# A gated linear attention in chunks with two dense layers: the alpha check per chunk, a reordered prologue, and TensorE's tile loop written out

## The reference, cut to what matters

```python
B, H, S, D = 4, 8, 768, 48
for t in range(S):                                  # per batch and head
    state = alpha[:, :, t, :, None] * state + k[t] (outer) v[t]
    y[:, :, t] = q[t] @ state                       # D x D state
x = y.transpose(0, 2, 1, 3).reshape(3072, 384)
x = (1 / (1 + exp(-(x @ w_gate))) * (x @ w_val)) @ w_out        # 384 -> 1536 -> 384
x = max(max(x @ w1, x @ w2), x @ w3) @ w_out2                   # 384 -> 768 -> 384
```

## Time and profile before

| what | us |
|---|---|
| median of 3 executions (892.06 to 894.14) | 893.74 |
| the profiled execution, its own time | 890.85 |
| its span, first to last instruction | 889.1 |
| TensorE busy in the span | 855.4 (96%) |
| VectorE, ScalarE, POOL busy | 413.7, 263.2, 120.8 |
| TensorE's mean granted clock | 0.989 |

### The profile page before, as it was taken

The page is one execution under the profiler, slowest core; times in us unless marked ns, Lnnn a source line. Parts: engine busy times, 40 slices in busy tenths (PEclk is TensorE's granted clock), DMA queues, the critical chain, the costliest instruction groups (busy, mean ns, idle before and its releaser), DMA issues.

```text
span 889.1 us, 13943 instructions
## 1 busy us (share of the span) xinstructions
PE 855.4 (96%) x5405; PEld 797.8 (90%) x5405; DVE 413.7 (47%) x730; ACT 263.2 (30%) x502; POOL 120.8 (14%) x95
## 2 busy tenths in 40 slices
PE   4599999999989999989999999999999999999997
PEld 3499999999989999989999999988888888888886
DVE  7888466366356456555546532232323222232321
ACT  3535333233232332232232233421212222121311
POOL 4355411011011111101101102510000000000000
PEclk9789999999999999999999999999999999999999
DMA  7481021021021021021021021300010000000000
GB/s 298 140 330 46 7 90 46 8 90 46 6 93 45 1 96 45 1 97 45 1 97 45 1 78 32 111 1 1 0 36 1 35 0 35 0 35 0 18 18 35
DMA packets 15603, 46.89 MB, mean 53 GB/s; under 512 B 2112, under 2 KB 6080, under 8 KB 15552
## 3 DMA queue, kind: packets, MB, share of 16 engines
q1 hardware_dynamic: 15552, 46.15, 14.7%
HBM read 40.24 MB, written 4.72 MB: 51 GB/s over the span
## 4 chain that ended last, share of the span: by engine, by line
PE 94%; DVE 2%; issue 1%; ACT 1%; DMA 1%; POOL 0%; SPq 0%; ACTq 0%; DVEq 0%; POOLq 0%
PE ps_gate L799 17%; PE ps_out L824 17%; PE ps_val L799 17%; PE ps_gate L805 8%; PE ps_val L805 8%; PE ps_out L896 6%; PE ps_sc L799 6%; PE ps_sc L805 3%; PE ps_sc L757 3%; PE ps_y L788 3%; PE ps_sc_odd L896 2%; PE ps_y L784 2%; PE ps_y L741 1%; PE ps_sc L767 1%; DVE rdec L566 1%
## 5 line engine op out<-in xcount | busy, mean ns | idle before, releaser
L799 PE MATMUL ps_gate<-x_hi,w_hi 128*128 128x384 f32 (+1 forms) x396 | 139.8, 353 | 7.2 <-issue 5.4
L799 PE MATMUL ps_val<-x_hi,w_hi 128*128 128x384 f32 (+1 forms) x396 | 140.7, 355 | 0.0
L799 PE MATMUL ps_gate<-x_hi,w_lo 128*128 128x384 f32 (+1 forms) x396 | 139.1, 351 | 0.0
L799 PE MATMUL ps_val<-x_hi,w_lo 128*128 128x384 f32 (+1 forms) x396 | 138.9, 351 | 0.0
L805 PE MATMUL ps_gate<-x_lo,w_hi 128*128 128x384 f32 (+1 forms) x396 | 118.1, 352 | 0.0
L629 DVE TENSOR_TENSOR h_sb<-act_sb,ps_val 128x384 f32<-128x384 f32 x96 | 52.7, 549 | 139.9 <-PE ps_val L805 139.8
L805 PE MATMUL ps_val<-x_lo,w_hi 128*128 128x384 f32 (+1 forms) x396 | 117.2, 350 | 0.0
L387 ACT ACTIVATE h_hi<-h_sb 128x384 fp32r<-128x384 f32 x96 | 50.4, 525 | 156.7 <-DVE h_sb L629 156.6
L428 ACT ACTIVATE act_sb<-ps_gate 128x384 f32<-128x384 f32 x96 | 47.2, 492 | 157.2 <-PE ps_gate L805 156.8
L714 DVE TENSOR_TENSOR probs<-probs,ps_val 128x512 f32<-128x512 f32 x36 | 24.7, 687 | 137.8 <-PE ps_val L805 137.8
L566 DVE RECIPROCAL rdec<-decay 112x128 f32<-112x128 f32 x96 | 85.7, 923 | 0.5
(11 more groups left out here) (98 smaller groups left out, 1245.7 us busy)
## 6 DMA issues: line engine op xcount, KB each, us to landing
inbuf<-att_in SPq DMA_DIRECT2D x23, 704.0 KB, 5.2
mid<-w SPq DMA_DIRECT2D x12, 576.0 KB, 9.3
inbuf<-att_in SPq DMA_DIRECT2D x23, 256.0 KB, 3.0
mid<-alpha_flat SPq DMA_DIRECT2D x8, 576.0 KB, 7.2
inbuf<-w SPq DMA_DIRECT2D x6, 768.0 KB, 4.3
out<-inbuf SPq DMA_DIRECT2D x5, 768.0 KB, 3.5
x_raw<-y_last SPq DMA_DIRECT2D x48, 24.0 KB, 1.9
out<-inbuf SPq DMA_DIRECT2D x4, 192.0 KB, 2.1
```

Of the source, the lines that this page charges most:

```text
L799: mm(bank, w_at(half, f, c + k * P, total=total), x_hi[:, k, 0:w], start=(k == 0 and half == 0), stop=False)
```

## The change

Every chunk's alpha is checked where it lies, after its scans, on ScalarE (two passes: |alpha - 1|, then relu(that - 0.25) with its row sum into a column of `viol`). The flag is made from the 24 columns in tile 7 and read by every engine after all its other work; the general path, now with both layers in it, follows there. `alpha_flat`, `distance`, `reduce_alpha`, the clamp, `finish_x` and its register are gone. `rdec` is no longer a reciprocal of `decay`: the last column is, and a second scan multiplies backwards from it by alpha. The prologue has another order on every engine. TensorE's loop over two tiles is written out as six tiles; the other engines keep theirs.

```diff
 def load_chunk(Cs, i):                                  # SP
     if isinstance(i, int) and Cs in (3, 4):
         sp.wait_ge(y_done, 5 - Cs)
+        sp.wait_ge(viol_done, 5 - Cs)
     elif not (isinstance(i, int) and Cs < 3):
         sp.wait_ge(u_done, Cs + 6 * i - 1)
+        sp.wait_ge(viol_done, Cs + 6 * i - 1)
...
+def load_w1(f):
+    if f >= RING:
+        sp.wait_ge(w_hi_done, f - RING + 1)
+        sp.wait_ge(w_lo_done, f - RING + 1)
+    elif f >= RING - 2:
+        sp.wait_ge(y_done, 3)
+        sp.wait_ge(viol_done, 3)
+    sp.dma_start(slot(f), w1[f]).then_inc(stage_in[f % RING], 16)
...
 load_chunk(0, 0)
+load_chunk(1, 0)
 sp.dma_start(cst[:, :], consts).then_inc(consts_in, 16)
-load_chunk(1, 0)
-load_ring(0)
-load_ring(1)
+load_w1(0)
 load_chunk(2, 0)
...
+for f in range(1, RING - 2):
+    load_w1(f)
+load_chunk(4, 0)
+load_chunk(3, 0)
+move_last(0, (0, 2))
+for f in range(RING - 2, NF1):
+    load_w1(f)
+load_chunk(5, 0)
+move_last(1)
```

POOL splits `w1[0]` in three parts, and TensorE's first gate and val product wait for a part each:

```diff
 scale_qk(0, 0)
 scale_qk(1, 0)
-split_w1(0)
+split_first(0).then_inc(w_lo_part, 1)
 scale_qk(2, 0)
-for f in range(1, NF1):
-    split_w1(f)
+split_first(1).then_inc(w_lo_part, 1)
+split_first(2).then_inc(w_lo_done, 1)
+for f in range(NF1):
+    if f > 0:
+        split_w1(f)
     if f in (2, 5, 8):
         scale_qk(CPT + (f - 2) // 3, 0)
```

ScalarE (`y_copy` now copies `y_last` first and signals it; `check` comes in every tile's f = 2, 5, 8 after h_hi):

```diff
+def check(Cs, i):
+    C = Cs + 6 * i
+    act.wait_ge(rdec_done, C * PAIRS + PAIRS)
+    a = buf_cols(buf(Cs), 0, PAIRS * CH)
+    nc.scalar.activation(a, a, ACT.Abs, bias=minus_one).then_inc(dist_done, 1)
+    act.wait_ge(dist_done, C + 1)
+    col = viol[:, bass.ds(C, 1)]
+    nc.scalar.activation(a, a, ACT.Relu, bias=minus_range, accum_out=col).then_inc(viol_done, 1)
...
+khs_copy(0, 0)
 split_w1(0)
-distance(0)
-khs_copy(0, 0)
-distance(1)
+act.wait_ge(consts_in, 16)
 y_copy(0, 0)
-distance(2)
 khs_copy(1, 0)
-split_w1(1)
-distance(3)
+check(0, 0)
+check(1, 0)
 y_copy(1, 0)
...
 y_copy(2, 0)
-for n in range(7, NA):
-    distance(n)
-split_w1(2)
+act.wait_ge(last_evac, CPT)
+for r in (0, ODD):
+    act.dma_start(x_raw[r + D:r + D + GAP, 1, :],
+                  y_last[r + GAP:r + 2 * GAP, :]).then_inc(last_moved[1], 16)
+khs_copy(2, 0)
+split_w1(1)
+act.wait_ge(y_evac, CPT)
 for k in range(KT):
     act.wait_ge(last_moved[k], 32)
     x_split(0, k, x_raw[:, k, :])
-act.wait_ge(flag_ready, 1)
-bad = act.value_load(flag_i[0:1, 0:1], min_val=0, max_val=1)
...
-layer1(0, 0, True, False, {f: (lambda f=f: split_w1(f + 3)) for f in range(NF1 - 3)})
+layer1(0, 0, True, False, {f: after_first_tile(f) for f in range(NF1 - 2)})
```

where `after_first_tile(f)` makes `check(2, 0)` at f = 0 and then `split_w1(f + 2)`. VectorE:

```diff
 def recips(Cs, i, pairs):
+    C, par = Cs + 6 * i, Cs % 2
+    if 0 in pairs:
+        dve.wait_ge(scan_done, C * PAIRS + PAIRS)
...
+        nc.vector.reciprocal(rdec[0:PR, par, :, CH - 1], decay[0:PR, par, :, CH - 1]).then_inc(rend_done, 1)
+        nc.vector.tensor_copy(d_end[0:PR, par, :], decay[0:PR, par, :, CH - 1]).then_inc(end_done, 1)
+        dve.wait_ge(rend_done, C + 1)
     for p in pairs:
-        nc.vector.reciprocal(rdec[0:PR, Cs % 2, p, :], decay[0:PR, Cs % 2, p, :]).then_inc(rdec_done, 1)
+        nc.vector.tensor_tensor_scan(rdec[0:PR, par, p, CH - 2::-1], att(buf(Cs), ALPHA)[:, p, CH - 1:0:-1],
+                                     zero[0:PR, :].broadcast_to([PR, CH - 1]), rdec[0:PR, par, p, CH - 1:CH],
+                                     ALU.mult, ALU.add).then_inc(rdec_done, 1)
...
-dve.wait_ge(consts_in, 16)
 scans(0, 0)
 recips(0, 0, range(PAIRS))
 scans(1, 0)
+recips(1, 0, range(PAIRS))
+dve.wait_ge(consts_in, 16)
 masked(0, 0, 0)
-recips(1, 0, (0,))
-reduce_alpha(0)
 masked(0, 0, 1)
-recips(1, 0, (1, 2, 3))
+scans(2, 0)
 dve.wait_ge(state_zero, 1)
 new_state(0, 0)
-scans(2, 0)
+recips(2, 0, range(PAIRS))
 masked(1, 0, 0)
 masked(1, 0, 1)
 new_state(1, 0)
 masked(2, 0, 0)
 masked(2, 0, 1)
+new_state(2, 0)
 for k in range(KT):
     x_rest(k, k, x_raw[:, k, :])
-new_state(2, 0)
```

TensorE (chunk 2 attends before its outer product, the constants are waited for only ahead of the first transposes):

```diff
-with pe.Fori(0, (TILES - 2) // 2) as i:
+for i in range((TILES - 2) // 2):
     for Ts in (1, 2):
-        layer1(Ts, i, True, True)
+        layer1(Ts, i, True, True, {})
-layer1(TILES - 1, 0, False, True)
+layer1(TILES - 1, 0, False, True, {3: flag_row})
```

More of the change, by code:

```diff
@@ L193, in build, with staged @@
         HALVES = (slice(0, D), slice(ODD, PR))
[L197 to L204, removed]
+        def staged(eng, f):
+            eng.wait_ge(stage_in[f % RING], 16 * (f // RING + 1))
         block = ctx.enter_context(nc.Block())
@@ L337, in _ @@
                 sp.dma_start(out[TILES2 - 1][:, s, :], stage_out[:, s, :]).then_inc(stored, 16)
+            with sp.If(bad):
+                sp.wait_ge(stored, 16 * (TILES2 - 1 + SUB))
+                general()
+                slow_layers()
             sp.wait_ge(stored, 16 * (TILES2 - 1 + SUB))
@@ L389, in split_w1 @@
             def split_w1(f):
[L390 to L391 removed]
+                staged(act, f)
+                copy(w_hi[:, f * W1C:(f + 1) * W1C], slot(f)).then_inc(w_hi_done, 1)
             def khs_copy(Cs, i):
@@ L407, in y_copy @@
                 for r in HALVES:
-                    copy(x_raw[r, :, t], ps_y[r, 0:KT, :])
-                for n, r in enumerate(HALVES):
                     ins = copy(y_last[r, t], ps_y[r, KT, :])
+                ins.then_inc(last_evac, 1)
+                for r in HALVES:
+                    ins = copy(x_raw[r, :, t], ps_y[r, 0:KT, :])
                 ins.then_inc(y_evac, 1)
@@ L485, in _, with after_first_tile, go @@
                 x_split(0, k, x_raw[:, k, :])
-            act.wait_ge(flag_ready, 1)
-            bad = act.value_load(flag_i[0:1, 0:1], min_val=0, max_val=1)
-            with act.If(bad):
-                general()
-                act.wait_ge(x_final, 1)
-                for k in range(KT):
-                    copy(x_hi[:, k, 0:TOK], x_raw[:, k, :]).then_inc(x_hi_redone, 1)
-            layer1(0, 0, True, False, {f: (lambda f=f: split_w1(f + 3)) for f in range(NF1 - 3)})
+            def after_first_tile(f):
+                def go():
+                    if f == 0:
+                        check(2, 0)
+                    split_w1(f + 2)
+                return go
+            layer1(0, 0, True, False, {f: after_first_tile(f) for f in range(NF1 - 2)})
             with act.Fori(0, (TILES - 2) // 2) as i:
@@ L540, in _ @@
             o_copy(TILES2 - 1)
+            act.wait_ge(flag_ready, 1)
+            bad = act.value_load(flag_i[0:1, 0:1], min_val=0, max_val=1)
+            with act.If(bad):
+                general()
+                slow_layers()
         @block.vector
@@ L689, in _ @@
-            dve.wait_ge(flag_step, 2)
-            nc.vector.tensor_scalar(flag_i[:, :], flag[:, :], ALPHA_RANGE, None, ALU.is_gt).then_inc(flag_ready, 1)
+            new_state(2, 0)
             for k in range(KT):
                 x_rest(k, k, x_raw[:, k, :])
-            new_state(2, 0)
-            dve.wait_ge(flag_ready, 1)
-            bad = dve.value_load(flag_i[0:1, 0:1], min_val=0, max_val=1)
-            with dve.If(bad):
-                general()
-                dve.wait_ge(x_final, 1)
-                dve.wait_ge(x_hi_redone, KT)
-                for k in range(KT):
-                    nc.vector.tensor_tensor(x_lo[:, k, 0:TOK], x_raw[:, k, :], x_hi[:, k, 0:TOK].bitcast(F32),
-                                            ALU.subtract).then_inc(x_lo_redone, 1)
@@ L727, in _ @@
             layer2(TILES2 - 1, True)
+            dve.wait_ge(flag_ready, 1)
+            bad = dve.value_load(flag_i[0:1, 0:1], min_val=0, max_val=1)
+            with dve.If(bad):
+                general()
+                slow_layers()
         @block.tensor
@@ L844, in layer1 @@
                         pe.wait_ge(h_done, g)
+                    if first and f == 0:
+                        pe.wait_ge(w_lo_part, 2)
                     product(ps_val[:, 0:TOK], f, DM, W1C).then_inc(val_done, 1)
@@ L932, in lay_out @@
+            pe.wait_ge(flag_ready, 1)
+            bad = pe.value_load(flag_i[0:1, 0:1], min_val=0, max_val=1)
+            with pe.If(bad):
+                general()
+                slow_layers()
 def lay_out(q, k, v, alpha, moe_w_gate, moe_w_val, moe_w_out, moe2_w1, moe2_w2, moe2_w3, moe2_w_out):
```

365 lines of the change are left out of this document (234 added, 131 removed).

## The result

The kernel after takes **881.61 us** (median of four executions, 880.59 to 882.18) against 893.61 (892.06 to 894.14, four executions) for the one before: a ratio of 0.9867, interval 0.985 to 0.9884, or 12.0 us. The forecast was 883.0. The profiled execution of after took 880.59 (span 878.8, granted clock 0.993) against 890.85 (889.1, 0.989) before, so it shows 10.3 of those 12.0 us; the experiments say where the rest is.

The account below looks back on a forecast made before the run. TensorE was taken as the bound from layer 1's first product on. The terms, 5.9 + 11.0 - 2.4 - 3.3 - 0.5 = 10.7 us saved, taken against the median 893.74, gave 883.0 us, range 876.5 to 889.

Parts of the forecast that it names:

- The loop written out: TensorE's layer-1 loop: writing it out removes two pauses at its backward jumps, 5.9 us saved, bounds 5.4 and 6.1.
- Start of layer 1: Prologue: the first product of layer 1 comes at 34 instead of 44.95, 11.0 us earlier.
- The 29: Prologue: attention ends at 29 us instead of 38.4, the middle between 31.3 and 26.5 for two TensorE clock rates.
- x_lo held: First lo pass of layer 1: POOL's w1[1] split holds VectorE's state operation and x_lo; 2.4 us lost, bounds 0 and 3.
- Tile 0: First tile of layer 1: TensorE waits for the later w1 splits and for k; 3.3 us lost, bounds 0 and 7.
- The end: Last tile and kernel end: the flag's transposition, reading it and jumping over a block; 0.5 us lost.
- the wait at f = 2: Tile 0, step f = 2: TensorE waits about 1.7 us for the chain of check, copy and POOL's split of w1[2].
- (a): Prologue and tile 0: the waits don't appear and TensorE is at full rate early; 876.3 us, chance 0.2.
- (b): Tile 0 is paced by POOL: w_lo a step late three times or the clock falls in a pause; 888.3, chance 0.17.
- (c): Tile boundaries still pause because ScalarE and DVE also jump; 888.9 us, chance 0.04.
- (e): Written-out tiles: straight-line code is not fetched in time, 2.7 us a tile; slower at 899.2 us, chance 0.04.
- (d): ScalarE reloads its tables between Sigmoid and Abs/Relu, 4.5 us more than the sum; 887.5 us, chance 0.04.

Follow-up runs that it names:

- rest_first: The kernel after with the three x_lo operations put ahead of chunk 2's state update on VectorE: 880.24 us.
- pool_waits: The kernel after with POOL's split of w1[1] held back until the three x_lo are made: 880.34 us.
- split_early: The kernel after with ScalarE's split of w1[2] and chunk 2's check ahead of tile 0, SP's w1[6] and w1[7] loads waiting for chunk 2's outer product: 880.17 us.
- no_jump: The kernel after without the general path at the end; engines still read the flag but have no block to jump over: 880.62 us.
- loop_back: The kernel after with TensorE's layer-1 loop over two tiles put back, nothing else: 890.66 us.
- after_again: The kernel after, unedited, run again beside the last group of follow-up runs: 881.73 us.
- pause_no_jump: The kernel after, loop still written out, with TensorE waiting at the start of tiles 3 and 5 for the next chunk's scans: 889.89 us.
- best: The kernel after with chunk 3's scans and products before tile 0, x_lo before state operations, POOL's splits behind x_lo, ScalarE's w1[1] and w1[2] splits behind x_hi: 877.1 us.
- before_no_check: The kernel before without the loads, passes and reductions over all of alpha, the flag made from zeros, weight loads moved up: 890.82 us.
- recip: The kernel after with rdec made by four reciprocals of decay again in place of the backward scans: 885.17 us.

## Why the prediction was right

The 883.0 is 1.4 above the measured 881.61, and the direction rests on the right mechanisms: an earlier start, no pauses, part of it given back in tile 0. But the loop's term was 3.1 us too small and the others together 1.8 too large; that the sum lies so near is in part luck.

- **The loop written out**, "I take 5.9 us, bounds 5.4 and 6.1": the pauses went, and in an execution whose clock holds they are worth 5.9. In medians the term is **9.0**. The step that failed is taking the pause's price from one profiled execution of before, in which the clock did not fall. The 2.9 us between that execution and the median were seen and carried over as a constant; in after the same difference is 1.0. The bounds did not allow for what follows a pause.
- **Start of layer 1**, 11.0 us earlier: 11.56. The attention ended at 28.97 (27.89 + 1.08) where 29 was predicted. The 29 was the middle between the two clocks, and it was met by luck: the other runs with this prologue end up to 1.5 us later (below). From there to the product are 4.4 us instead of 4.95: ScalarE issued its two DMAs beside its own copies (its queue's entries at 29.61 and 30.27, its copies at 29.60 and 30.10), where the sum laid them end to end.
- **x_lo held**, 2.4: 2.24. rest_first, pool_waits and split_early bear out the reason, DVE and POOL taking turns also on the small state operations.
- **Tile 0**, 3.3 (its four parts add up to 3.2): the wait at f = 2 was 1.87 (1.7 predicted), the one for k 0.47 (0.9), and at f = 5 and 8 there was none (0.3 each). The check took 1.6 us, not 1.2. Together with x_lo's these waits are 4.6 of the 5.4 that tile 0 lost; the other 0.8 wasn't traced to a cause; three drains and restarts would make most of it, at the 0.25 us by which each pause cost more than its idle time (5.9 against 5.4 for two).
- **The end**, 0.5: 1.64 in the profile, of which no_jump takes away 1.6. It was costed by "0 to 1.5 us" and taken too low.
- **Rivals**: (a) fell with the waits, (b) with the waits at f = 5 and 8, (c) and (e) with the boundaries, which show no pause, (d) with the one table load.

In medians: 9.0 from the loop, 3.0 from all the rest, against a forecast of 5.9 and 4.8. The rest shows 4.5 in the profiled executions (11.56 - 5.4 - 1.64), but 3.0 in the medians. Part of that is the start, which varies: in the runs whose prologue is that of after, the first product stands at 33.39 (after), 33.68 (loop_back), 34.17 (after_again), 34.24 (pause_no_jump), 34.72 (no_jump) and 34.89 (pool_waits). It follows when TensorE reaches its faster pace in the scores of chunk 2. One matmul of that group from the timeline of after, and one from that of pool_waits:

```profile
24.50 0.27 PE L849 MATMUL ps_sc<-mid 48*128 48x128 f32 x1
```

```profile
25.46 0.42 PE L851 MATMUL ps_sc<-mid 48*128 48x128 f32 x1
```

In after all but the first pair of them take 0.27 us, in after_again the first four are slower, in pool_waits all take 0.42 or more. The profiled execution of after had the earliest start of the six and was the fastest of its four, so its differences flatter the change. For what is left between 4.5 and 3.0 no run gives a cause.

## What to carry to other kernels

A pause on TensorE costs its own length and, in part of the executions, the clock behind it: where a kernel's times scatter and its granted clock varies, look for pauses of two to three us, and price an edit that removes one against the median of both kernels, not from a single trace. Where VectorE and POOL share a critical stretch, moving POOL's work moves only who is held; put it where VectorE reads PSUM or is idle, as best did. When a pass is taken out of a prologue, ask first (before_no_check is the case here) whether the order of the steps behind it, and not the pass, sets the start.

## What was not expected of the hardware

- Two pauses of one execution, much alike, can end differently: in pause_no_jump both waits are 2.87 us (products at 248.52 and 387.79), and only the second is followed by the lower clock; in loop_back 2.93 us (at 247.98) is not and 3.24 is. Shorter waits differ in the same way: 1.88 us in rest_first is followed by it, 1.87 in after and 2.46 in pool_waits are not. The length alone does not decide it here; what does stays open.
- VectorE's copy of 112x4 elements (`d_end`) took 0.14 us with POOL idle and 1.19 beside POOL's q product, though it reads one tensor; its timeline in after:

```profile
398.01 0.18 DVE L626 RECIPROCAL rdec<-decay 112x4 f32<-112x4 f32 x1 [0.20 <-DVE decay L616]
398.11 1.19 DVE L627 COPY d_end<-decay 112x4 f32<-112x4 f32 x1
```

  Reciprocals kept their length (925 ns on the mean in recip, 923 before), and so did `h_sb`, which reads one side from PSUM (0.55 us at 45.82 in after, inside POOL's split of 45.53). Over the kernel the 24 copies cost 23.2 us of VectorE, nearly all of it beside a busy TensorE.
- The row sum of an activation is an instruction of its own on ScalarE, 0.186 us each.
- A taken jump over a long block at the very end costs 1.6 us in the trace, though SP's wait for the last stores stands behind it.
